# The second head's turned probabilities: VectorE in place of ScalarE empties their PSUM bank

## The reference, cut to what matters

```python
for e in range(4):                                   # experts, 64 wide each
    q = x @ wq[e]; k = x @ wk[e]; v = x @ wv[e]
    scores = scale * (q @ k.transpose(0, 2, 1))      # causal: 576 x 576
    scores = np.where(causal, -1e9, scores)
    a = np.exp(scores - scores.max(-1, keepdims=True))
    a /= a.sum(-1, keepdims=True) + 1e-09
    ye = a @ v @ wo[e]
    out += gate[..., e] * ye                         # top 2 of 4
```

## Time and profile before

| | |
|---|---|
| median of 3 runs | 872.27 us (870.17 to 872.38) |
| profiled execution, its own time | 872.52 us |
| its span, first to last instruction | 870.7 us |
| busy: TensorE matmul, weight load | 841.0 us (97%), 738.5 us (85%) |
| busy: VectorE, ScalarE, GpSimd | 460.5 us, 403.4 us, 189.7 us |
| the copies of the turned probabilities, L652 | 160 on ScalarE, 63.5 us, mean 455 ns |
| the same kind on VectorE, L918 | 32, 128x256 only |

### The profile page before, as it was taken

The page is one execution under the profiler, slowest core; times in us unless marked ns, Lnnn a source line. Parts: engine busy times, 40 slices in busy tenths (PEclk is TensorE's granted clock), DMA queues, the critical chain, the costliest instruction groups (busy, mean ns, idle before and its releaser), DMA issues.

```text
span 870.7 us, 17273 instructions
## 1 busy us (share of the span) xinstructions
PE 841.0 (97%) x6717; PEld 738.5 (85%) x6717; DVE 460.5 (53%) x1345; ACT 403.4 (46%) x979; POOL 189.7 (22%) x236
## 2 busy tenths in 40 slices
PE   6898999999999999999999999999999999999898
PEld 4586898978989798988989789897988889897796
DVE  1457655466444655466543765446554565546630
ACT  0448623475134832466324762348323673247521
POOL 1403233002330133202330032401332013310320
PEclk9889999999999999999999999999999999999999
DMA  9910345003050032300341012500304000100001
GB/s 276 232 26 2 110 110 110 13 2 107 4 115 2 1 111 51 71 2 2 110 77 38 2 54 57 122 2 2 110 25 92 1 2 2 43 25 2 2 1 61
DMA packets 117408, 47.32 MB, mean 54 GB/s; under 512 B 94352, under 2 KB 110736, under 8 KB 117328
## 3 DMA queue, kind: packets, MB, share of 16 engines
q1 hardware_dynamic: 117328, 46.21, 21.3%
HBM read 35.19 MB, written 9.44 MB: 51 GB/s over the span
## 4 chain that ended last, share of the span: by engine, by line
PE 84%; DVE 9%; ACT 2%; SPq 2%; issue 1%; DMA 1%; POOL 0%; DVEq 0%; ACTq 0%
PE w L982 35%; PE t L982 22%; PE t L1029 6%; PE w L1013 6%; PE t L1045 5%; PE t L1141 3%; PE w L1195 2%; PE t L1149 2%; DVE w L770 2%; DVE big L817 1%; PE t L1059 1%; ACT probs L637 1%; DVE work L937 1%; DVE work L945 1%; DVE work L918 1%
## 5 line engine op out<-in xcount | busy, mean ns | idle before, releaser
L982 PE MATMUL t<-big,wqk_s 128*128 128x288 f32 x768 | 111.5, 301 | 2.9 <-DVE big L875 1.7
L982 PE MATMUL w<-wout_s,big 128*128 128x512 f32 x432 | 108.1, 399 | 1.5 <-DVE big L817 0.6
L982 PEld LDWEIGHTS t<-big,wqk_s 128*128 128x128 f32 x768 | 104.4, 190 | 4.1 <-issue 2.4
L982 PE MATMUL w<-wsgT_s,big 128*128 128x288 f32 x768 | 107.6, 296 | 0.0
L982 PEld LDWEIGHTS w<-wsgT_s,big 128*128 128x128 f32 x768 | 104.2, 189 | 0.0
L637 ACT ACTIVATE probs<-w,neg_max 128x64 f32<-128x64 f32 (+4 forms) x160 | 83.1, 526 | 38.3 <-DVE neg_max L770 35.6
L982 PEld LDWEIGHTS w<-wout_s,big 128*128 128x128 f32 x432 | 79.6, 188 | 20.3 <-DVE big L817 3.2
L541 POOL TENSOR_TENSOR yT<-squares,yT 128x256 fp32r<-128x256 f32 (+1 forms) x32 | 22.4, 699 | 309.9 <-ACT yT L671 309.9
L770 DVE CUSTOM_DVE_ANT_0 w<-w,causal 128x64 f32<-128x64 f32 (+4 forms) x160 | 75.4, 513 | 19.3 <-PE w L1013 18.2
L652 ACT ACTIVATE work<-t 128x384 f32<-128x384 f32 (+3 forms) x160 | 63.5, 455 | 31.0 <-PE t L1029 29.5
L685 ACT ACTIVATE big<-work 128x576 fp32r<-128x576 f32 x32 | 22.0, 687 | 111.9 <-POOL work L560 96.3
(11 more groups left out here) (114 smaller groups left out, 1400.2 us busy)
## 6 DMA issues: line engine op xcount, KB each, us to landing
kin<-in_k_dram SPq DMA_DIRECT2D x8, 1024.0 KB, 6.2
vin<-in_v_dram SPq DMA_DIRECT2D x8, 1024.0 KB, 8.6
out_dram<-work SPq DMA_DIRECT2D x32, 256.0 KB, 2.1
qin<-in_q_dram SPq DMA_DIRECT2D x112, 72.0 KB, 2.4
staged_win<-in_moe_w_in_dram SPq DMA_DIRECT2D x4, 512.0 KB, 6.2
staged<-in_moe_w_sg_dram SPq DMA_DIRECT2D x4, 288.0 KB, 4.0
kin<-in_k_dram SPq DMA_DIRECT2D x8, 128.0 KB, 2.8
vin<-in_v_dram SPq DMA_DIRECT2D x8, 128.0 KB, 6.7
```

The source lines that it names most:

```text
L982: last = nc.tensor.matmul(o, stationary(hs, c), mv(hm, c), start=c == of[0] and p == 0, stop=c == of[-1] and p == len(PASSES) - 1)
```

## The change

The head 0 copy of each step stays on ScalarE. The head 1 copy of the first part (`t`) goes to VectorE, at the same place of the list; the waits that step 0 needs go with it. 80 of the 160 copies move.

```diff
                     elif kind == "t":            # in the ScalarE program
                         lo, hi = T_GROUPS[j // 2][0]
-                        for a in range(2):
-                            V = ("t", j, a, 0)
-                            x = src(V)
-                            if j == 0 and a == 0:
-                                for r in range(2):
-                                    act.wait_ge(stored[r], stored_at[part, "t"][r] if part > 0 else 16)
-                                if part == 0:
-                                    act.wait_ge(wo_lo, 1)
-                            give(nc.scalar.activation(pT[:, j % 2, a, P * lo:P * hi], x[:, 0:P * (hi - lo)],
-                                                      ACT.Copy), V)
+                        V = ("t", j, 0, 0)
+                        x = src(V)
+                        if j == 0:
+                            for r in range(2):
+                                act.wait_ge(stored[r], stored_at[part, "t"][r] if part > 0 else 16)
+                            if part == 0:
+                                act.wait_ge(wo_lo, 1)
+                        give(nc.scalar.activation(pT[:, j % 2, 0, P * lo:P * hi], x[:, 0:P * (hi - lo)], ACT.Copy), V)
...
+                    elif kind == "t":            # in the VectorE program, ahead of "t2"
+                        lo, hi = T_GROUPS[j // 2][0]
+                        V = ("t", j, 1, 0)
+                        x = src(V)
+                        if j == 0:
+                            for r in range(2):
+                                dve.wait_ge(stored[r], stored_at[part, "t"][r] if part > 0 else 16)
+                            if part == 0:
+                                dve.wait_ge(wo_lo, 1)
+                        give(nc.vector.tensor_copy(pT[:, j % 2, 1, P * lo:P * hi], x[:, 0:P * (hi - lo)]), V)
```

## The result

The kernel after took 875.28 us, the median of 9 runs (873.66 to 878.02), against 870.99 us before (869.82 to 874.34, 9 runs). The ratio is 1.0048, 95% interval 1.0029 to 1.0066: slower by 0.5%, where 0.46% was forecast. The absolute times are less close than that: the forecast of 876.3 us started from 872.27, the median of the first 3 runs before, and the 9 runs give 1.3 us less. The profiled execution took 877.37 us, its span 875.6.

A forecast was written before the change was run, and what follows sets the result against it. TensorE was taken as the bound, with almost no slack. Waits of 3 x 0.82 + 4 x 0.46 - 0.3 = 4.0 us, added to the profiled 872.52 and set against the median, gave 876.3 us, 0.46% slower; range 872.5 to 879.0.

The forecast's parts named there:

- The bound, and no gain from ScalarE: Whole kernel: TensorE's matmuls cover 97% of the span; ScalarE's 403 us bound nothing by themselves.
- The copies' cost: The 80 moved copies on VectorE: 287, 419, 551 or 683 ns each, 40 us more in all.
- Step 2's copy hidden, ScalarE's relief of 0.27 us: `t` 2's copy makes no TensorE wait; step 4's exponentials start 0.27 us sooner, VectorE is 0.27 us early for step 5's maxima.
- Step 3's copy exposed: Head 1 of step 4's transposes: TensorE waits for `t` 3's copy, 0.82 us in even, 0.46 us in odd batches.
- L781 held by GpSimd in even batches: Step 4's scaling row: GpSimd's L541 still holds this VectorE instruction, which ends at 285.96 us; not held in odd batches.
- rival 2: Step 4's scaling row: L781 gets ahead of L541, so even batches wait 0.46 us like odd; 875.2 us; chance 10%.
- Later copies covered: Copies of `t` 4 to `t` 9: no second wait; in even batches `t` 4's counts on TensorE's 0.82 us lag.
- Nothing takes the wait back: TensorE's 0.46 us wait before L1059 moves along with TensorE, so the full 0.82 or 0.46 us reaches the end.
- rival 3: TensorE's wait before L1059 shrinks by its lateness; even batches lose 0.36 us, odd none; 873.1 us; chance 17%.
- Batch 0: L911, for which TensorE waits twice there, comes about 0.31 us forward; -0.3 us, counted once.
- rival 1: ScalarE's relief doesn't reach L911; step 4's transposes wait 1.07 us (even) and 0.72 us (odd); 878.4 us; chance 17%.
- Rival 4: VectorE is fed earlier in all batches, each gaining 0.31 us; 869.8 us, not slower; chance 8%.

The follow-up runs named there:

- e3: Kernel after, with VectorE doing the moved copies of steps 0 to 5 ahead of the same step's scaling row; 871.35 us, ratio 1.0000 to before.
- e6: Kernel before, with one semaphore instruction put on VectorE behind the gate ranks of the last tile; 869.05 us, one run.
- e2: Kernel before, with only step 3's head 1 copy moved to VectorE (8 of 160 copies); 877.52 us, ratio 1.0075 to before.
- e4: Kernel after, with GpSimd's low part of tile 0 (L541) made to wait until step 4's scaling row is done; 874.71 us, one run.
- e1: Kernel after, with only step 3's head 1 copy back on ScalarE (72 of 80 stay moved); 871.35 us, ratio 1.0006 to before.
- e7: Kernel before, with VectorE doing step 7's scaling row ahead of step 8's maxima; 866.58 us, ratio 0.9949 to before.

## Why the prediction was right

- **The bound, and no gain from ScalarE.** Right. 22 us less work on ScalarE shortened nothing by itself: ScalarE's idle time before the exponentials rose from 38.3 to 48.8 us, and with the wait for the scaling row at 0.59 us in both, the stretch is 612.40 us with the 80 copies on VectorE (e3) as with all on ScalarE (e6).
- **The copies' cost.** 287, 419, 551, 683 ns estimated; 283, 417, 551, 685 measured. VectorE has 37.1 us more (40 forecast). ScalarE was to end near 367 us and is at 381.4: the forecast took off 80 copies at their mean of 455 ns, but two in a row overlap (0.66 us for a pair of 0.40 us each), and the copies' own busy time fell by 27.4 us, from 63.5 to 36.1. Where the other 5.4 us went stays open; nothing in the sum used that figure.
- **Step 2's copy hidden, ScalarE's relief of 0.27 us.** Right; L909 comes 0.23 us earlier against the start of batch 2, and e2 takes the relief away: the waits grow from 0.42 and 0.78 to 0.69 and 1.03.
- **Step 3's copy exposed.** Right in place and nearly in size: 0.46 and 0.82 forecast for what TensorE is late, 0.42 and 0.78 of idle time shown. Against the start of its batch, TensorE is 0.44 and 0.78 us late at the next transposes, those of step 5 (batches 1 and 2).
- **L781 held by GpSimd in even batches.** Right (0.52 us); rival 2 did not come, and e4 shows what it would have brought: 0.34 us in each even batch.
- **Later copies covered.** Right for the kernel as it is, by TensorE's lateness for step 4's copy, as the sum had it: in even batches e1 shows 0.33 us once that lateness is gone.
- **Nothing takes the wait back.** Wrong by 0.1 us a batch. The wait before L1059 was to stay at 0.46 us on the matmuls and is 0.35; its shrinking was even named as a sign of being wrong, and that sign came. But it shrank not by absorbing, as rival 3 has it: e6 gets the same 0.1 us with no copy moved.
- **Batch 0.** -0.3 forecast, -0.26 read. The first of the two waits for L911 fell from 1.11 to 0.88 us, the second did not change, as the sum had it. That no copy would make TensorE wait there was wrong, at no cost: the wait of 0.61 us at step 1.
- **The sum.** 4.0 forecast. The traces give -0.26 + 2.97 for batches 0 to 6 and 0.42 - 0.1 for batch 7: 3.0 us. The term that was too large is the net loss a batch: 0.33 and 0.66 against 0.46 and 0.82. Of the 1.0 us that this makes, 0.7 is the 0.1 us of the scaling row in seven batches, the rest the waits' own size. The medians differ by 4.3 us, with an interval of 2.5 to 5.7; the 1.3 us between is inside it. The two profiled spans differ by 4.9: to the 3.0 come a start-up 2.5 us later and an end (behind the last copy's start, where the last store lies) 0.8 us longer after, and one stage of batch 7 that ran 1.5 us slower before:

```profile
823.12 7.86 PE w L982 x48
```

  Its like in batch 7 after takes 6.39. TensorE's granted clock was 0.80 in those 7.86 us, and 1.00 in the 6.39. The nearness of forecast and median is thus partly luck.
- **Rivals 1 and 4.** e2 is rival 1 made on purpose, and isn't what happened. Rival 4 would need TensorE waiting for L911 in batches 1 to 7: no such wait is in the trace after.

## What to carry to other kernels

Before work is moved from a half-idle engine to another half-idle one, ask of each piece when its output slot is wanted next, and what stands ahead of it in the new queue: here one copy in ten decided, and its place in the queue (e3) was worth as much as the whole change. The path of that copy runs through ScalarE too, so the relief made the wait 0.27 us shorter (e2), but could not take it away. A new wait can cover a second one behind it, so an experiment that removes the first should be read for the next. And where the bound engine waits for another that had been idle just before, reorder there first: a few lines (e7) gave 0.5%, which moving 80 copies could not.

## What the runs showed of the hardware

- At the one place tried, with two waits back to back ahead of a VectorE instruction, it began 0.1 us later on its release than with a semaphore instruction between them; TensorE's wait behind it was 0.69 in place of 0.59 us (before against e6).
- A two-column instruction on VectorE took 0.51 to 0.61 us beside a GpSimd instruction of 0.73 us (before, after, e1), and 0.16 us when the latter was put behind it (e4); a copy out of PSUM that lay wholly inside the same GpSimd instruction kept its 0.42 us (e3).
- One stage took 7.86 us at a granted clock of 0.80, and 6.39 us at 1.00 (batch 7, before and after).
